# Router steps of an attention-and-expert kernel dealt out anew around each pair's last scan, with its GpSimd adds, attention gate and last pair reordered

## The reference

```python
scores = where(causal, -1e9, scale * q @ k.T);  a = softmax(scores)
local = a @ v                                   # per head: 576 x 64
q_p = where(q > 0, q, exp(q) - 1) + 1           # = max(q, 0) + min(exp(q), 1)
mem_out = (q_p @ M_prev) / (q_p @ z_prev + 1e-6)
g = 1 / (1 + exp(-beta))                        # one per head
x = g * mem_out + (1 - g) * local
e_idx = argmax(x @ w_gate)                      # the token's expert
gate_w = softmax(x @ w_gate)[e_idx];  eom = sigmoid(x @ w_output_gate)[e_idx]
out = gate_w * eom * (relu(x @ w1[e]) @ w2[e])  # for the tokens of expert e
```

## Time and profile before

| | us |
|---|---|
| median of 3 runs (lowest, highest) | 495.48 (494.32, 498.02) |
| the profiled execution | 495.07 |
| its span | 493.3 |
| PE busy in the span | 467.3 (95%) |
| DVE busy | 312.9 (63%) |
| ACT busy | 279.8 (57%) |
| POOL busy | 197.0 (40%) |
| PE's share of the chain that ended last | 75% |
| DVE's share of it | 11% |

### The profile page before, as it was taken

One profiled execution on the slowest core, in us unless ns is written; L12 is line 12 of the kernel. 1 busy time (PEld: TensorE's weight loads), 2 busy tenths in 40 slices (PEclk: granted clock), 3 DMA queues, 4 the chain that ended last, 5 costly groups with the idle time before them and its releaser, 6 DMA issues.

```text
span 493.3 us, 11147 instructions
## 1 busy us (share of the span) xinstructions
PE 467.3 (95%) x3920; PEld 377.3 (76%) x3921; DVE 312.9 (63%) x785; ACT 279.8 (57%) x623; POOL 197.0 (40%) x187
## 2 busy tenths in 40 slices
PE   5999999989998998998999999999999999999995
PEld 4777777767776775886888887888888788878884
DVE  5597889988987997794222279822223983982221
ACT  5678877888896786435222248522224864862221
POOL 6457665688897768225223101121111012021100
PEclk9899999999998998999999999999999999999999
DMA  6333444395342552248221166940111694630000
GB/s 200 102 99 100 128 123 126 116 353 175 100 126 86 152 165 69 72 154 276 64 65 64 43 219 224 323 183 22 43 43 58 223 328 175 204 150 21 21 14 22
DMA packets 47359, 64.54 MB, mean 131 GB/s; under 512 B 9678, under 2 KB 28622, under 8 KB 47312
## 3 DMA queue, kind: packets, MB, share of 16 engines
q1 hardware_dynamic: 43232, 54.34, 34.3%
q0 software_dynamic: 4080, 9.60, 6.0%
HBM read 57.03 MB, written 10.90 MB: 138 GB/s over the span
## 4 chain that ended last, share of the span: by engine, by line
PE 75%; DVE 11%; issue 5%; DMA 4%; SPq 3%; ACT 1%; DVEq 1%; POOL 0%; ACTq 0%; POOLq 0%
PE O_ps L1516 8%; PE S L1516 8%; PE O_ps L1518 8%; PE S L1518 8%; PE O_ps L1517 8%; PE S L1517 8%; PE O_ps L1348 8%; PE S L1348 7%; PE TP_ps L1543 4%; DVE probs L913 3%; PE STK L1348 3%; PE TP_ps L1348 2%; DMA v_nat<-in_v 2%; PE STK L1507 2%; PE TP_ps L1344 2%
## 5 line engine op out<-in xcount | busy, mean ns | idle before, releaser
L1213 DVE TENSOR_TENSOR hid_lo<-TP_ps,hid_hi 128x512 fp32r<-128x512 f32 x46 | 31.8, 691 | 109.2 <-ACT hid_hi L828 97.0
L724 ACT ACTIVATE probs<-probs,neg_max 128x128 f32<-128x128 f32 (+2 forms) x144 | 82.8, 578 | 13.9 <-DVE neg_max L913 13.5
L672 POOL DMA_INDIRECT out<-x_ring,slot_tok_i x23 | 24.2, 1051 | 144.4 <-ACT x_ring L836 125.1
L1516 PE MATMUL S<-w_hi,x_hi 128*128 128x512 f32 x180 | 72.3, 402 | 0.0
L1518 PE MATMUL S<-w_hi,x_lo 128*128 128x512 f32 x180 | 70.4, 391 | 0.0
L1517 PE MATMUL S<-w_lo,x_hi 128*128 128x512 f32 x180 | 70.2, 390 | 0.0
L599 POOL DMA_INDIRECT x_ring<-x_tokens,slot_tok_i x28 | 31.2, 1115 | 82.4 <-DMA out<-x_ring,slot_tok_i 71.0
L1516 PE MATMUL O_ps<-w_hi0b,hid_hi 128*128 128x512 f32 x152 | 62.8, 413 | 1.2 <-DVE hid_lo L1213 0.9
L1518 PE MATMUL O_ps<-w_hi0b,hid_lo 128*128 128x512 f32 x152 | 59.5, 391 | 0.0
L1348 PE MATMUL S<-k_pair,q_pair 64*128 64x128 f32 (+3 forms) x224 | 48.4, 457 | 11.7 <-DVE neg_max L913 8.2
L1517 PE MATMUL O_ps<-w_lo0b,hid_hi 128*128 128x512 f32 x152 | 59.4, 391 | 0.0
(11 more groups left out here) (232 smaller groups left out, 957.2 us busy)
## 6 DMA issues: line engine op xcount, KB each, us to landing
w_raw<-in_moe_w SPq DMA_DIRECT2D x60, 512.0 KB, 5.6
q_pair<-in_qt SPq DMA_DIRECT2D x15, 288.0 KB, 2.8
k_pair<-in_kt SPq DMA_DIRECT2D x15, 288.0 KB, 3.1
v_nat<-in_v SPq DMA_DIRECT2D x16, 256.0 KB, 3.1
x_tokens<-x_out SPq DMA_DIRECT2D x16, 256.0 KB, 2.4
x_ring<-in_moe_w SPq DMA_DIRECT2D x3, 512.0 KB, 8.1
m_aug<-in_m_aug SPq DMA_DIRECT2D x1, 648.0 KB, 5.5
q_tail<-in_qt SPq DMA_DIRECT2D x32, 16.0 KB, 2.9
```

Of the source, the lines that this page charges most:

```text
L672: nc.gpsimd.indirect_dma_start(out=out[:, :], out_offset=bass.IndirectOffsetOnAxis(ap=slot_tok_i[:, t:t + 1], axis=0), in_=x_ring[:, t % X ...
L724: last = nc.scalar.activation(pr, pr, ACT.Exp, bias=neg_max[:, slot, h:h + 1], scale=-1.0, accum_out=sums[g % 2][:, at:at + 1])
L1213: V.tensor_tensor(hid_lo[:, 4 * f:4 * f + 4, :], TPB_ps[:, f, :].rearrange("r (c t) -> r c t", c=4), hid_hi[:, 4 * f:4 * f + 4, :].bitcast ...
L1516: T.matmul(dst, hi, part(i, k)[:, cols], start=first, stop=False)
```

## The change

1. The router's table is dealt out anew, in shorter pieces: `choose` loses its first two operations to a new `largest`, `order` its first to `read_counts`, `place` its first to `read_ranks`, and `startup_rest` becomes `turning_weights`, `router_consts` and `token_digits` in pairs 1, 2 and 3. `routing_behind` now comes before the copy `unload(g, 3)`, and `rank` moves to pairs 8, 11 and 13 (in 13 behind all the transposes). ACT's `route_exps` and SP's `store_scale` follow.
2. On POOL, `positive` and the minimum stand together (`phi_parts`), `lanes` runs before the `phi_T` add, and that add waits until PE has made the first score rows of the next pair. `low_ahead` moves to pairs 10, 11, 13 and 15, ahead of `phi_parts`; SP waits for each such piece where it waited for all.
3. The local branch's gate is multiplied into `turn_w` once; `dens` becomes an add with one operand.
4. In pair 15, `early_table` stands ahead of two transposes, the exponentials of the last scan ahead of a copy on ACT, and `local(14)` ahead of the last transposes; `early_tiles` is done in pair 14. After pair 15, DVE waits for `phi_pos` before it splits weights.

The core of the diff:

```diff
-    RANK_PAIR = {7: 0, 10: 1, 14: 2}
-    READS = {6: 1, 7: 2, 10: 3, 14: 4}
+    RANK_PAIR = {8: 0, 11: 1, LAST * NPAIR + 1: 2}
+    READS = {6: 1, 8: 2, 11: 3, LAST * NPAIR + 1: 4}
+    LOW_PAIR = {10: 0, 11: 1, 13: 2, 15: 3}
...
-                    if g == (10, 14, 15)[b]:
+                    if g == (10, 12, 15)[b]:
                         store_scale(b)
-                if g == G - 2:
-                    sp.wait_ge(lo_first, KD)
+                if g >= G - 2:
                     x = expert_at(1)
-                    for k in range(KD):
+                    for k in {G - 2: range(KD - 1), G - 1: (KD - 1,)}.get(g, ()):
+                        sp.wait_ge(lo_first, k + 1)
...
-            def positive(g):
+            def phi_parts(g):
                 if not valid(g):
                     return
                 pool.wait_ge(ld_first, 32)
                 pool.wait_ge(ld_qk[g % 2], 64 * uses(g))
                 wait(pool, phi_done, g)
                 nc.gpsimd.tensor_scalar(q_pos[:, :], q_pair[g % 2][:, :], 0.0, None, ALU.max).then_inc(phi_pos, 1)
+                pool.wait_ge(phi_exp, g + 1)
+                nc.gpsimd.tensor_scalar(q_exp[:, :], q_exp[:, :], 1.0, None, ALU.min).then_inc(phi_pos, 1)
             def phi(g):
                 if not valid(g):
                     return
-                pool.wait_ge(phi_exp, g + 1)
-                nc.gpsimd.tensor_scalar(q_exp[:, :], q_exp[:, :], 1.0, None, ALU.min).then_inc(phi_pos, 1)
                 pool.wait_ge(phi_pos, 2 * (g + 1))
+                if valid(g + 1):
+                    pool.wait_ge(scored, NS * (g + 1) + len(SLOTS[0]))
                 wait(pool, mem_mm, g - 1)
                 nc.gpsimd.tensor_tensor(phi_T[g % 2][:, 0:S], q_exp[:, :], q_pos[:, :], ALU.add).then_inc(phi_done, 1)
...
-                positive(g)
...
-                phi(g)
-                for b in range(LAST):
-                    if g == (8, 13, 14)[b]:
-                        lanes(b)
-                if 0 <= g - 9 < KD:
-                    low_ahead(g - 9)
+                if g in LOW_PAIR:
+                    low_ahead(LOW_PAIR[g])
...
+                phi_parts(g)
+                for b in range(LAST):
+                    if g == (9, 12, 14)[b]:
+                        lanes(b)
+                phi(g)
...
-                    if g == (8, 12, 14)[b]:
+                for b in range(2):
+                    if g == (8, 10)[b]:
                         route_exps(b)
                 unload(g, 2)
-                unload(g, 3)
-                exps(g, 7)
+                if g == G - 1:
+                    exps(g, 7)
+                    unload(g, 3)
+                else:
+                    unload(g, 3)
+                    exps(g, 7)
+                if g == LAST * NPAIR + 1:
+                    route_exps(2)
...
-                V.tensor_copy(turn_w[:, :, D:HC], w_pair[:, :, :])
+                dve.wait_ge(consts_dve, 3)
+                V.reciprocal(gate_loc[:, 1, :], gate_loc[:, 0, :]).then_inc(consts_dve, 1)
+                dve.wait_ge(consts_dve, 4)
                 for h in range(2):
                     half = slice(h * D, (h + 1) * D)
-                    last = V.tensor_copy(turn_w[half, :, 0:D], ident[half, None, half].broadcast_to([D, NPAIR, D]))
+                    gate = gate_loc[half, 1, h:H:2][:, :, None]
+                    V.tensor_tensor(turn_w[half, :, D:HC], w_pair[half, :, :], gate.broadcast_to([D, NPAIR, RE]), ALU.mult)
+                    last = V.tensor_tensor(turn_w[half, :, 0:D], ident[half, None, half].broadcast_to([D, NPAIR, D]),
+                                           gate.broadcast_to([D, NPAIR, D]), ALU.mult)
                 last.then_inc(consts_dve, 1)
...
-                V.scalar_tensor_tensor(dens[:, :], sums[u][:, :], 1e-9, gate_loc[:, p, :], ALU.add, ALU.mult).then_inc(summed, 1)
+                V.tensor_scalar(dens[:, :], sums[u][:, :], 1e-9, None, ALU.add).then_inc(summed, 1)
...
             def routing_ahead(g):
-                if g == 7:
-                    experts_in_order()
+                if g == 1:
+                    turning_weights()
+                elif g == 2:
+                    router_consts()
+                elif g == 3:
+                    token_digits()
+                elif g == 5:
+                    largest(0)
+                    choose(0)
+                elif g == 7:
+                    order()
                 elif g == 8:
+                    open_gate(0)
+                    order_rest()
+                    so_far(1, 1)
+                elif g == 9:
                     scale(0)
-                elif g == 12:
-                    scale(1)
-                elif g == 13:
-                    choose(2)
-                elif g == 14:
-                    scale(2)
-                elif g == 15:
-                    early_tiles()
-            def routing_behind(g):
-                if g == 5:
-                    choose(0)
-                    so_far(0, 1).then_inc(first_hot, 1)
-                elif g == 6:
-                    order()
-                elif g == 7:
                     place(0)
-                    open_gate(0)
-                elif g == 9:
+                elif g == 10:
                     choose(1)
-                    so_far(1, 1).then_inc(hot_done, 1)
-                elif g == 10:
-                    place(1)
                     open_gate(1)
                 elif g == 11:
                     so_far(1, 2)
+                    scale(1)
+                elif g == 12:
+                    place(1)
                 elif g == 13:
+                    largest(2)
+                    choose(2)
                     so_far(2, 3).then_inc(hot_done, 1)
+                elif g == 14:
+                    scale(2)
+                    place(2)
+            def routing_behind(g):
+                if g == 5:
+                    so_far(0, 1).then_inc(first_hot, 1)
+                elif g == 6:
+                    read_counts()
+                elif g == 7:
+                    experts_in_order()
+                elif g == 8:
+                    read_ranks(0)
+                elif g == 9:
+                    largest(1)
+                elif g == 11:
+                    read_ranks(1)
+                elif g == 13:
                     open_gate(2)
-                    order_rest()
                 elif g == 14:
-                    place(2)
+                    early_tiles()
...
+                    dve.wait_ge(phi_pos, 2 * G - 1)
...
                     mask_row(g, 7)
+                    routing_behind(g)
                     if g == G - 1:
                         early_tokens()
                         unload(g, 2)
                     unload(g, 3)
-                    routing_behind(g)
+                    if RANK_PAIR.get(g) == 2:
+                        read_ranks(2)
...
                 tail_scores(g)
+                if g == G - 1:
+                    early_table()
                 for back, k in LATE:
                     turn(g, k)
-                    if g == G - 1 and (back, k) == LATE[0]:
-                        early_table()
+                if RANK_PAIR.get(g) == 2:
+                    pe.wait_ge(masked, NS * (g + 1))
+                    rank(2)
+            local(G - 2)
             turn(G - 1, NU - 1)
-            local(G - 2)
             values(G - 1)
```

53 lines of the change are left out of this document (27 added, 26 removed).

## The result

The changed kernel took 517.84 us (median of 4 runs, 516.92 to 519.55) against 496.75 us (494.32 to 498.41) for the kernel before on the same chip: a ratio of 1.043, interval 1.038 to 1.049. It is 21 us slower; the forecast was 506.5 us, within 499 to 511. The direction was right and the size was not. The ratios leave out slower executions that some kernels had (once 2585.16 us, in d_ahead_load), and one trace is of such an execution, that of a_pool_before: 502.22 us, where seven of its twelve took 494.1 to 497.5.

The account below looks back on a forecast made before the run. PE, busy 95% of the span, was taken as the bound. From 495.07 us, -12.5 + 13.5 + 1.6 + 0.7 + 2.2 + 5.1 + 0.8 = +11.4 gave 506.5 us, range 499 to 511.

Parts of the forecast that it names:

- Removed, -12.5: V(1) to V(15): short pieces and the moved phi_T add take away the whole excess over undisturbed distances, -12.5 us.
- The wait of 0.90 per pair, +13.5: Memory products in 15 pairs: PE waits 0.90 us for a phi_T add that itself waits for PE, +13.5 us.
- the rival "faster": Memory products: phi_T is ready by the end of local, so no wait and no shifted load, 485.6 us; chance 0.08.
- Long pieces, +1.6: Ahead of the last scan: router pieces over the 1.09 us of room in pairs 5, 7, 8, 11, 13, 14.
- remaining collisions, +0.7: Pairs 10, 11 and 13: pieces meet POOL's one-operand work pushed back by the weight subtraction, between 0 and 1.8 us.
- Lanes, +2.2: Pairs 12 and 14: lanes ahead of the phi_T add make it 0.85 and 1.35 us late.
- The values' load, +5.1: Pair 8's values' load ends 3.6 us later, delaying V(9): +3.4, and 1.7 for a low clock behind.
- The rival without it (501.4): Values' load of pair 8 is not late, so the 5.1 us drop out: 501.4 us; chance 0.2.
- The start, +0.9: First pair: the same 0.90 us wait for phi_T as in the other pairs, counted within the +13.5.
- The end, +0.8: Pair 15: 1.5 us sooner start, then about 2.5 us wait behind early gathers; between -1 and +2.5 us.
- The rule and the row: DVE beside POOL: the skill's full exclusion against a row where one-operand POOL work costs a start up to 0.4 us.
- the rule's 509: Pairs 10, 11, 13: full exclusion makes DVE wait out POOL's one-operand work, +2.8 us, total 509; chance 0.07.

Follow-up runs that it names:

- d_ahead_load: d_ahead with SP's q and k loads waiting for the last operation reading their buffer, not for the addition: 493.97 us, ratio 0.992.
- a_pool_before: The changed kernel without the add's wait, POOL's work in the order of before, weight subtractions in steps 10, 11, 12 and 13: 497.43 us, ratio 0.997.
- a_no_gate: The changed kernel without the phi_T add's wait for the next pair's first score rows: 512.03 us, ratio 1.030.
- b_gate: The kernel before with only the phi_T add's wait for the next pair's first score rows added: 529.38 us, ratio 1.067.
- a_gate_tail: The changed kernel with one number edited: the phi_T add waits for its own pair's last score products, not the next pair's first: 507.14 us, ratio 1.019.
- a_gate_from_1: The changed kernel with the add's wait only from pair 1 on, so pair 0's add does not wait for score rows: 512.28 us, ratio 1.028.
- d_ahead: c_all with the phi_T add also waiting until DVE has finished the pieces ahead of the last scan: 497.97 us, ratio 0.998.
- a_v_first: The changed kernel with the values' load of pair 8 issued ahead of the eight weight pieces: 514.6 us, ratio 1.039.
- a_load_early: The changed kernel with SP's q and k loads waiting for the last operation reading their buffer, not for the addition: 513.77 us, ratio 1.033.
- a_gathers_behind: The changed kernel with the two early gathers issued behind the phi_T add of pair 15: 508.96 us, ratio 1.023.
- e_low_behind: d_ahead_load with the weight subtractions of steps 10, 11 and 13 behind the phi_T add: 489.26 us, ratio 0.984.
- b_gate_weights: The kernel before with only the gate moved into the turning weights and dens a one-input operation: 497.96 us, ratio 1.001.
- c_all: a_gate_tail with lanes and early gathers behind the phi_T add: 499.86 us, ratio 1.003.

## Why the prediction was right and wrong

- **Removed, -12.5: right in direction.** Collisions with two-operand work ahead of the scan are gone in the changed kernel, and last-scan waits are at most 0.7. `dens` is not 0.16 everywhere, but 0.16 to 0.45. a_no_gate and b_gate show that this holds only with the new position of the addition *and* the new place of the pieces.
- **The wait of 0.90 per pair, +13.5: right.** The undisturbed distance is 11.48 as 10.58 + 0.90; a_no_gate restored 10.58. Its parts show in the undisturbed pair: the memory products start at V + 7.68 instead of V + 6.86, and 0.08 is lost behind them. The 0.82 is the 0.62 of the sum and two handshakes of 0.14 (from the score rows to the addition) and 0.06 (from its end to PE), where 0.28 was taken. The row's 0.62 of idle time is smaller than 0.82 because it counts from the end of `local`, which the memory products used to overlap by 0.20. But the rival "faster", held improbable by plain arithmetic, was one number away: a_gate_tail has most of the protection with no wait in undisturbed pairs.
- **Long pieces, +1.6, and remaining collisions, +0.7: right within what can be told.** In the changed kernel pairs 5, 7, 10 and 11 cost 0.3 to 0.5 each over 11.48, and pair 13 1.0. Pairs 1 and 4, booked at nothing, cost 0.3 and 0.4. In pair 4 the addition starts 0.4 later behind the score rows than elsewhere, in every kernel with the condition but a_gate_from_1; the profile shows no reason, and this stays open. With nothing else in the way (d_ahead) pairs 3, 5 and 7 wait 0.29, 0.77 and 0.51 where I had 0, 0.08 and 0.3.
- **Lanes, +2.2: the waits were right, the consequence was mis-sized.** 1.67 and 2.02 against 0.62 are 1.05 and 1.40 (forecast 0.85 and 1.35). Behind the second the clock fell: 198 to 200 ran at 0.50, and V(15) - V(14) is 14.59 where 13.1 was booked. I added a low clock for the load's gap of 3.4, and none for gaps of about 2, though the kernel before had shown one behind a gap of 2.17. The length of the gap alone doesn't settle it: behind pair 12's 1.67 there was none in the changed kernel, and 1.6 us of it in a_v_first and a_load_early. So such a gap needs a price with a chance, not a price or nothing.
- **The values' load, +5.1: right.** The wait was 3.70 (3.4 forecast), the two distances held 5.6 over 11.48; a_load_early shows the named cause, `phi_done`. The rival without it (501.4) falls.
- **The start, +0.9 booked inside the 13.5: wrong by 4.4.** I priced the first pair like the others. There POOL's addition waits for PE with nothing else of POOL ahead, PE waits 1.65, and the clock falls behind it: 2.9 in all (a_gate_from_1). Of the other 2.4 us, 1.6 are the router-weight products, which vary from run to run, 0.4 their later begin, and 0.4 stays open.
- **The end, +0.8: wrong by 3.6.** `phi_T` came at V(15) + 14.7 (13.6 to 14.5 forecast), so the place was nearly right; the addition took 2.40 instead of 1.41. The term held a wait of 2.5 (3.63 measured), but the sentence "may lower the clock again" was not priced: 214 to 224 at 0.50 to 0.55. a_gathers_behind puts the whole at 7.0, against a gain of 2.6 beneath.
- **The rule and the row.** One-operand POOL work beside DVE took at most 0.55 from an operation of DVE and not the rest of its 1.65; the rule's 509 is nearer to the total, but for another reason. But the prediction's reading, that the start costs up to 0.4 and the rest runs alongside, holds only for operations with two SBUF inputs, such as the `expert_i` of its row. In e_low_behind the one-input `dens` began 1.03 after `q_pos` and ended with it, and in the changed kernel the 0.45 of pair 10 is the same. For two-operand POOL work the Trainium skill's rule (SBUF — State Buffer, on the two separate sides) and the runs agree for operations with two SBUF inputs. It says the same of the two-port modes, and `dens` with one input is held to the end just as long: 1.09 to 1.38 in b_gate_weights.

In one sentence: each mechanism was named, and the sum was short because gaps of 1.65 to 3.63 us on PE were priced at their length, while three of them (start, pair 14, end) cost a further 1.6, 1.5 and 3.4 us by PE's clock. That is 6.5 of the 11.4 us missed. Another 2.4 are the rest of the late start, and the others are small excesses of several terms.

## What to carry to other kernels

When a condition makes one engine wait, ask for the earliest event that gives nearly the same protection: here "own last scores" instead of "next first scores" was 10.7 us. Price a gap on PE twice, without and with the low clock that this kernel's own traces show behind some gaps of that length, and give each a chance. Look at the first and the last pair by themselves, since nothing covers them there. And cut a buffer's release to its last reader: the loads waited for an operation that never read the buffer, and it cost 4 us in two kernels. An edit that helps in one variant (lanes behind, 9.2) can be worth nothing in the next, because what it pushes back collides there.

## What the runs showed of the hardware

- One-input DVE operations on SBUF (`dens`, `digits`, a cast) that begin beside a two-operand POOL operation are held until its end as surely as two-input ones, also with 5 to 20 elements per partition: 0.17 became 1.27, 2.35 at most. Reciprocals (at most 0.22), reductions (0.16 to 0.38) and the 128x576 scans with a PSUM input (0.74 to 0.76) never were.
- Beside a one-operand POOL operation of 1.65 us (`q_pos`, `q_exp`) it depends on when the DVE operation begins, in all 17 traces alike. Begun in the first half microsecond, it ended about 0.7 after the POOL operation's start (`expert_i`, two inputs, took 0.60 and ended 0.68 after it; `dens` at 114.76 in c_all, one input, took 0.67 and ended 0.71 after it). Begun from 0.6 to 0.9, it was undisturbed (`dens` 0.16 in pairs 3, 11 and 13 of the changed kernel). Begun from 1.0 to 1.4, one-input operations were held to the end (`dens` in e_low_behind) and two-input ones were not (`r_hot` in pair 10 of the changed kernel: 0.20, begun at 1.14).
- It goes the other way too: the addition took 2.40 instead of 1.41 beside DVE's two-input `w_lo0b`.
- Behind the 3.63 us gap at the end the granted clock stayed at the 1.2 GHz level for 8 us and more, although PE was busy without a break (8.00 of 8.00 us); in the middle of the kernel, behind gaps of 2 to 3.7 us, it was about 3 us. What makes the difference stays open.
